# Attention's lead-in, first iteration and drain in orders of their own, 0/1 matrices by large instructions, and experts and last stage in one block

## The reference

```python
def _attn_ref(r, k, v, w, a, b) -> np.ndarray:
    B, H, S, D = r.shape
    state = np.zeros((B, H, D, D), dtype=np.float32)
    y = np.zeros_like(r)
    for t in range(S):
        ...
        y[:, :, t] = np.einsum('bhd,bhde->bhe', rt, state)
        Sa = np.einsum('bhde,bhe->bhd', state, at)
        state_decay = state * wt[:, :, None, :] - np.einsum('bhd,bhe->bhde', Sa, bt)
        state = state_decay + np.einsum('bhd,bhe->bhde', vt, kt)
    return y.astype(np.float32)

def _moe_ref(x, w_gate, w_noise, noise, w1, w2) -> np.ndarray:
    ...
    noisy_logits = logits + noise_scale * noise
    top2 = np.argpartition(-noisy_logits, 2, axis=1)[:, :2]
    ...
            h = np.maximum(x[mask] @ w1[e], 0.0)
            out[mask] += top2_w[mask, k, None] * (h @ w2[e])
    return out.astype(np.float32)

def _moe2_ref(x, w_in, w_out) -> np.ndarray:
    h = x @ w_in
    sp = np.where(h > 20.0, h, np.log1p(np.exp(np.minimum(h, 20.0))))
    g = h * np.tanh(sp)
    return (g @ w_out).astype(np.float32)
```

## Time and profile before

| | us |
|---|---|
| median of 3 runs (1692.13 to 1694.26) | 1694.13 |
| the profiled execution, whole | 1690.76 |
| its span | 1689.0 |

### The profile page before, as it was taken

One profiled execution on the slowest core, in us unless ns is written; L12 is line 12 of the kernel. 1 busy time (PEld: TensorE's weight loads), 2 busy tenths in 40 slices (PEclk: granted clock), 3 DMA queues, 4 the chain that ended last, 5 costly groups with the idle time before them and its releaser, 6 DMA issues. The chain is left out here.

```text
span 1689.0 us, 43070 instructions
## 1 busy us (share of the span) xinstructions
PE 1474.6 (87%) x18793; PEld 1138.5 (67%) x18793; DVE 597.6 (35%) x1198; ACT 575.3 (34%) x1137; POOL 326.6 (19%) x311
## 2 busy tenths in 40 slices
PE   0687897988989772699999999999858999999999
PEld 0577787877878661588888888888624555555556
DVE  8563653636544317000000000000027455454441
ACT  0453543525435310111111121212117545545541
POOL 5433222232321005311111111111041010000000
PEclk9877978969778755799999999999969999999999
DMA  3324133241321107555555555555161010000000
GB/s 85 81 52 112 39 87 70 53 114 38 90 67 27 43 19 251 181 186 164 187 164 185 167 179 172 173 175 171 45 196 30 24 31 28 24 28 9 8 12 20
DMA packets 99896, 159.88 MB, mean 95 GB/s; under 512 B 54464, under 2 KB 68800, under 8 KB 98432
## 3 DMA queue, kind: packets, MB, share of 16 engines
q1 hardware_dynamic: 92128, 131.23, 26.5%
q0 software_dynamic: 7584, 25.90, 5.0%
HBM read 140.21 MB, written 16.88 MB: 93 GB/s over the span
## 5 line engine op out<-in xcount | busy, mean ns | idle before, releaser
L951 PE MATMUL pY<-down,hT 128*128 x880 | 245.9, 433 | 0.0
L932 PEld LDWEIGHTS pH<-exT,up 128*128 128x128 f32 x1760 | 206.5, 193 | 11.5 <-issue 1.7
L1097 PE MATMUL mpY<-wout,h 128*128 128x320 f32 x768 | 210.4, 433 | 0.0
L932 PE MATMUL pH<-exT,up 128*128 128x128 f32 x1760 | 207.0, 276 | 2.5 <-ACT exT L971 1.5
L987 DVE COPY ys<-pY 128x320 f32<-128x320 f32 x55 | 27.0, 492 | 505.9 <-PE pY L951 505.9
L951 PEld LDWEIGHTS pY<-down,hT 128*128 128x128 f32 x880 | 163.0, 190 | 61.2
L978 ACT ACTIVATE hT<-pH 128x512 f32<-128x512 f32 x110 | 59.7, 594 | 418.0 <-PE pH L937 418.0
L1097 PEld LDWEIGHTS mpY<-wout,h 128*128 128x128 f32 x768 | 144.3, 190 | 60.7 <-issue 3.0
L1084 PE MATMUL mpH<-mxT,win 128*128 128x512 f32 x384 | 174.0, 607 | 4.9 <-ACT mxT L1126 4.1
L1084 PEld LDWEIGHTS mpH<-mxT,win 128*128 128x128 f32 x384 | 74.4, 195 | 92.6 <-issue 84.2
L1134 ACT ACTIVATE act_in<-act_in 128x512 f32<-128x512 f32 x96 | 59.9, 629 | 184.0 <-DVE act_in L1173 184.0
(11 more groups left out here) (179 smaller groups left out, 2196.8 us busy)
## 6 DMA issues: line engine op xcount, KB each, us to landing
up<-in_moe_w SPq DMA_DIRECT2D x55, 1024.0 KB
up_rest<-in_moe_w SPq DMA_DIRECT2D x110, 128.0 KB
down<-in_moe_w SPq DMA_DIRECT2D x8, 1280.0 KB, 14.6
results<-ys POOLq DMA_DIRECT2D x55, 160.0 KB
wfr<-in_wdec SPq DMA_DIRECT2D x16, 480.0 KB
kbT<-in_kb SPq DMA_DIRECT2D x16, 480.0 KB
uv<-in_vt SPq DMA_DIRECT2D x16, 240.0 KB, 6.2
aT<-in_at SPq DMA_DIRECT2D x16, 240.0 KB
```

What stands on the lines that cost most here:

```text
L932: pe.matmul(pH[t % 2][b][:, c, :], up[t % NU][:, k, f * P:(f + 1) * P], xT[t % 2][:, k, :], start=(c == 0 and k == 0), stop=False, skip_gr ...
L951: m = pe.matmul(pY[t % 2][:, 0:D], hT[t % 2][:, j, :], down[:, bass.ds(e, 1), j, :].rearrange("q n d -> q (n d)"), start=(j == 0), stop=(j ...
L1097: m = pe.matmul(pY[t % 2][:, 0:D], h[g % 2][:, f, j * P:(j + 1) * P], wout[:, f, :], start=(f == 0), stop=(f == FT - 1))
```

## The change

- In attention the list is chosen by iteration: LEAD in iteration 0, ORDER in 1 to 7, DRAIN in 8, SECOND_HALF in 9. LEAD begins with p0 and has the decays of group 1 (p0, p1), K, T, M and B at other places; DRAIN has the same operations as were left of ORDER, at other places between the hops.
- At the start VectorE clears `wfr` in two halves, makes the masks before the decays, and scales one half of group 0's `aT` and `kbT`, GpSimd the other; ScalarE clears the PSUM tiles. `wfr` is loaded in halves, each with its semaphore, and v of group 0 behind `kbT`.
- In routing VectorE marks tiles and rows with six large instructions in bf16, and ScalarE weights the tile matrix (2 large and 24 small instructions); GpSimd's 48 products and VectorE's 96 small instructions go.
- `experts` and `mish_ffn` return what each engine does, and `build` runs both in one block. The last stage's tiles `h` and two of `act_in` lie in the room of the down weights, its PSUM tiles are those of the experts, and its weights have room of their own. Its bodies are otherwise the same.

```diff
+
+LEAD = """p0 N0 K1 N1 K0 T0 M1 T1 n2_0 M0 n2_1 B0 t2_0 t2_1 w2_1 n4_0 w2_0 p1 n4_1 B1 t4_1 t4_0 V1 n8_0 w4_0 t8_1 t8_0
+w8_0 n8_1 n16_0 w4_1 n16_1 w16_0 w8_1 V0 L0 w16_1 E0 E1 L1 F0 F1""".split()
+DRAIN = """u s ST1 r u s r u UT1 s r H1 u s r u s r u s r u s I1 r J1 Y1 u UT0 s r H0 u X1 s r u ST0 s I0 r J0 Y0 u s
+X0 r u""".split()
 CHAIN = ("u", "s", "r")
 FIRST_HALF = ("UT0", "ST0", "H0", "I0", "J0", "Y0", "X0")
-SECOND_HALF = ("UT1", "ST1", "H1", "I1", "J1", "Y1", "X1")
+SECOND_HALF = ("ST1", "UT1", "H1", "I1", "J1", "Y1", "X1")
...
 
+    def order_of(it):
+        return LEAD if it == 0 else ORDER if it < GR else DRAIN if it == GR else SECOND_HALF
+
...
+        def scale_a(unit, eng, g, i):
+
+            eng.wait_ge(a_loaded, (g + 1) * 32)
+            eng.wait_ge(decayed, 2 * g + i + 1)
+            unit.tensor_tensor(aT[g % 3][:, i, :], aT[g % 3][:, i, :], dec[g % 3][i][:], ALU.mult).then_inc(a_scaled, 1)
+
+        def scale_kb(unit, eng, g, i):
+
+            eng.wait_ge(kb_loaded, (g + 1) * 32)
+            eng.wait_ge(decayed, 2 * g + i + 1)
+            backwards = after[i][:, ::-1].rearrange("q (c f) -> q c f", f=C).unsqueeze(2).to_broadcast([P, NC, 2, C])
+            unit.tensor_tensor(kbT[:, i], kbT[:, i], backwards, ALU.mult).then_inc(kb_scaled, 1)
+
         block = ctx.enter_context(nc.Block())
 
         @block.sync
         def _(sp):
-            def load_decays(g):
+            def load_decays(g, i):
                 for h in range(2):
-                    sp.dma_start(wfr[64 * h:64 * h + D], wdec[g, h]).then_inc(w_loaded, 16)
+                    sp.dma_start(wfr[64 * h:64 * h + D, i], wdec[g, h][:, i]).then_inc(w_loaded[i], 16)
...
 
-            sp.wait_ge(w_pads, 1)
-            load_decays(0)
-            load_v(0)
+            for i in range(2):
+                sp.wait_ge(w_pads, i + 1)
+                load_decays(0, i)
             sp.wait_ge(pads_set, 1)
             load_a(0)
             sp.wait_ge(pads_set, 2)
             load_kb(0)
+            load_v(0)
             sp.dma_start(gw[:], gate_w).then_inc(gate_loaded, 16)
             sp.wait_ge(pads_set, 3)
             for it in range(GR + 2):
                 g = it + 1
                 if g < GR:
-                    sp.wait_ge(decayed, 2 * it + 2)
-                    load_decays(g)
+                    for i in range(2):
+                        sp.wait_ge(decayed, 2 * it + i + 1)
+                        load_decays(g, i)
                 if 1 <= it <= GR:
                     if it >= 2:
...
+            act.wait_ge(zeros, 1)
+            for t in (*slot, chain):
+                m = copy(t[:].rearrange("q i w -> q (i w)"), st[:].rearrange("q c i f -> q (c i f)")[:, 0:2 * 512])
+            m.then_inc(cleared, 1)
             for it in range(GR + 2):
                 hop = 0
-                for tok in ORDER:
+                for tok in order_of(it):
...
             def make_decays(g, i):
-                dve.wait_ge(w_loaded, (g + 1) * 32)
...
-            nc.vector.memset(wfr[:], 1.0).then_inc(w_pads, 1)
-            for t in (mark, mark_r, st):
-                nc.vector.memset(t[:], 0.0)
-            for t in (*slot, chain):
-                m = nc.vector.memset(t[:], 0.0)
-            m.then_inc(cleared, 1)
-            dve.wait_ge(cleared, 1)
+            for i in range(2):
+                nc.vector.memset(wfr[:, i], 1.0).then_inc(w_pads, 1)
+            nc.vector.memset(st[:], 0.0).then_inc(zeros, 1)
+            nc.vector.memset(mark[:], 0.0)
+            after_step(nc.vector.memset(mark_r[:], 0.0))
             after_step(nc.vector.memset(mark_r[:, 0::C], 1.0))
-            make_decays(0, 0)
-            make_decays(0, 1)
             dve.wait_ge(const, 2)
             nc.vector.tensor_copy(identh[:], ident[:])
             for lo in (0, 64):
@@ -647,9 +658,15 @@
             dve.wait_ge(masked, 1)
             nc.vector.tensor_scalar(mask_un[:], mask_u[:], -1.0, None, ALU.mult).then_inc(masked, 1)
             dve.wait_ge(masked, 2)
+            make_decays(0, 0)
+            make_decays(0, 1)
+
+            dve.wait_ge(decayed, 2)
+            scale_a(nc.vector, dve, 0, 1)
+            scale_kb(nc.vector, dve, 0, 1)
             for it in range(GR + 2):
                 hop = 0
-                for tok in ORDER:
+                for tok in order_of(it):
                     if tok in ("p0", "p1"):
...
-            for j in range(2 * T):
-                nc.gpsimd.tensor_scalar(tile_hot[:, j, 1, :], minus_m[:], minus_tile[:, j // 2, j % 2:j % 2 + 1], row_of[:],
-                                        ALU.is_equal, ALU.mult).then_inc(by_pool, 1)
+            nc.gpsimd.tensor_copy(iota_rowh[:], iota_row[:])
+            nc.gpsimd.tensor_copy(minus_mh[:], minus_m[:]).then_inc(const, 1)
...
             for j in range(2 * T):
-                pe.wait_ge(by_dve, j + 1)
-                pe.wait_ge(by_pool, j + 1)
+                if j % QUARTER == 0:
+                    pe.wait_ge(in_row, j // QUARTER + 1)
+                if j % 2 == 0:
+
+                    pe.wait_ge(weighted, j // HALF + j // 2 + 2)
...
             nc.scalar.activation(gsum[:], gap[:], ACT.Exp).then_inc(soft, 1)
+            for half in range(2):
+                js = slice(half * HALF, (half + 1) * HALF)
+                act.wait_ge(in_tile, half + 1)
+                nc.scalar.activation(tile_hot[:, js, 1, :], tile_one[:, js, :], ACT.Copy, scale=row_of[:]).then_inc(weighted, 1)
+                for t in range(half * HALF // 2, (half + 1) * HALF // 2):
+                    nc.scalar.activation(tile_hot[:, 2 * t:2 * t + 2, 0, :], tile_one[:, 2 * t:2 * t + 2, :], ACT.Copy, scale=float(t)).then_inc(weighted, 1)
 
         @block.vector
...
             then(vec.scalar_tensor_tensor(minus_tile[:], row[:], 0.0, tile_f[:], ALU.is_lt, ALU.subtract))
-            vec.scalar_tensor_tensor(row[:], minus_tile[:], float(P), posf[:], ALU.mult, ALU.add).then_inc(split_up, 1)
-            dve.wait_ge(split_up, 1)
-            for j in range(2 * T):
-                vec.tensor_scalar(tile_hot[:, j, 0, :], minus_m[:], minus_tile[:, j // 2, j % 2:j % 2 + 1], float(j // 2), ALU.is_equal, ALU.mult)
-                vec.tensor_scalar(row_hot[:, j, :], iota_row[:], row[:, j // 2, j % 2:j % 2 + 1], None, ALU.is_equal).then_inc(by_dve, 1)
+            then(vec.scalar_tensor_tensor(row[:], minus_tile[:], float(P), posf[:], ALU.mult, ALU.add))
+
+            def mark_tiles(half):
+                js = slice(half * HALF, (half + 1) * HALF)
+                vec.tensor_tensor(tile_one[:, js, :], minus_mh[:].unsqueeze(1).to_broadcast([P, HALF, M]),
+                                  minus_tile[:].rearrange("q t k -> q (t k)")[:, js].unsqueeze(2).to_broadcast([P, HALF, M]), ALU.is_equal).then_inc(in_tile, 1)
+
+            def mark_rows(quarter):
+                js = slice(quarter * QUARTER, (quarter + 1) * QUARTER)
+                vec.tensor_tensor(row_hot[:, js, :], iota_rowh[:].unsqueeze(1).to_broadcast([P, QUARTER, P]),
+                                  row[:].rearrange("q t k -> q (t k)")[:, js].unsqueeze(2).to_broadcast([P, QUARTER, P]), ALU.is_equal).then_inc(in_row, 1)
+
+            mark_tiles(0)
+            mark_rows(0)
+            mark_tiles(1)
+            for quarter in range(1, 4):
+                mark_rows(quarter)
             then(vec.tensor_copy(pos[:].rearrange("q (t k) -> q t k", k=2), posf[:]))
...
 
-def experts(nc, x, results, w1, down, down_loaded, tile_expert, slot_token, ident):
...
+    return (load, gather, multiply, activate, combine), y_copied, pX, [p for tile in pH for p in tile], pY
...
+def mish_ffn(nc, ctx, results, results_copied, last, w_in, w_out, out, pos, gates, ident, room, pX, pH, pY):
...
+
+    GATE, ROWS = GT * GT * P, FT * GT * P
+    act_in = [room[:, 2 * ROWS + i * GATE:2 * ROWS + (i + 1) * GATE].rearrange("q (f n) -> q f n", n=GT * P) for i in range(2)]
+    act_in.append(sb("act_in", [P, GT, GT * P])[:])
+    h = [room[:, i * ROWS:(i + 1) * ROWS].rearrange("q (f n) -> q f n", n=GT * P) for i in range(2)]
+    pH = [p[:].rearrange("q c f -> q (c f)") for p in pH]
...
+                pe.wait_ge(wout_loaded, 16)
+                pe.wait_ge(results_copied, last)
...
         route(nc, logits, moe_noise, pos, gates, tile_expert, slot_token, ident, load_down)
-        experts(nc, x, results, moe_w1, down, down_loaded, tile_expert, slot_token, ident)
-        stage.close()
-        mish_ffn(nc, results, moe2_w_in, moe2_w_out, out, pos, gates, ident)
+        run_experts, results_copied, pX, pH, pY = experts(nc, stage, x, results, moe_w1, down, down_loaded, tile_expert, slot_token, ident)
+        run_ffn = mish_ffn(nc, stage, results, results_copied, M, moe2_w_in, moe2_w_out, out, pos, gates, ident,
+                           down[:].rearrange("q e t d -> q (e t d)"), pX, pH, pY)
+        block = stage.enter_context(nc.Block())
+
+        @block.sync
+        def _(sp):
+            run_experts[0](sp)
+            run_ffn[0](sp)
```

(20 more changed lines are left out.)

592 lines of the change are left out of this document (283 added, 309 removed).

## The result

The changed kernel takes 1655.59 us (median of 4 runs, 1650.57 to 1660.92) where the kernel before takes 1693.13 (4 runs beside it, 1691.86 to 1694.26): 37.5 us faster by the medians. The forecast was 1652.5 with a range of 1640 to 1664. The total was right; of its four terms two were right (routing and seam), the one for the lead-in was wrong, and the drain's is within the scatter.

What follows compares the result with a forecast made beforehand. Experts and last stage were taken as full on TensorE, so gains lie where TensorE waits: -13.3 (start and lead-in) + 3.4 (drain) - 18.9 (routing) - 12.8 (seam) = -41.6; 1694.1 - 41.6 = 1652.5 us, range 1640 to 1664.

Steps and rivals of the forecast that it cites:

- Start: Kernel start: kbT scaled at 25.6 us, first matmul 13 us sooner, but N0's mask only at 39.5 (before 40.28).
- Lead-in: Attention's iteration 0: first matmul of iteration 1 at 72.2 us, 13.3 us gained; bounds 9 and 17.
- B1 filled at 56.1: Lead-in: B1 filled at 56.1 us, then 16.1 us until kbT of group 1 is loaded and scaled, giving 72.2.
- F1 done at 66: Lead-in: at roughly 1 us per operation F1 is done at 66 us, before group 1's kbT at 72.2.
- Drain: Attention's drain: new order takes 55.1 us where 51.7 stood, 3.4 us lost; bounds 8 gained and 7 lost.
- never full, 7 lost: Drain's lower bound: if the granted clock is never full, the new order loses 7 us.
- Routing: Routing: inverse read at 664.7 us instead of 683.58 with matrices made by VectorE and ScalarE; 18.9 us gained.
- Rival 3: Routing: 0/1 matrices made slowly, broadcast operand at 2.1 ns per element; kernel at 1662 us; chance 0.07.
- Seam: Between experts and last stage: 12.8 us gained, 9.4 from the block's end and 3.4 from gathers not sharing queues.
- Rival 2: Seam: the wait stays because the stores' completion, not the block, took 9 us; kernel at 1661 us; chance 0.10.
- the first matmul near 72: Sign that the forecast is right: first matmul of attention's iteration 1 comes near 72 us.
- an iteration period off 70.5 by over 1.5 us: Sign that the forecast is wrong: attention's iterations differ from 70.5 us by over 1.5 us.

Runs made afterwards that it cites:

- late_loads: Changed kernel, but SyncE issues the loads of iteration 1 only behind N1 of group 1; 1649.0 us, ratio 0.9690 to the kernel before.
- route_only: Kernel before with only the new making of the routing's 0/1 matrices; 1678.38 us, ratio 0.9889.
- early_late_filler: Changed kernel with group 1's decays loaded before the clears' wait, iteration 1's loads behind N1, four unused matmuls behind each drain hop; 1633.56 us.

## Why the prediction was right, and where it was not

1. **Start.** Right by mechanism: the first matmul at 26.9 (25.6), p0 ahead of N0's mask, held by its load, that by the clears. The mask came at 40.74, forecast 39.5. The load took 4.7 us from issue where I had 5.2, but kbT was in at 21.7 where I had 20.5, and GpSimd's half of it took 4.99 beside VectorE's instruction where this chain had 3.4.
2. **Lead-in: the step that failed.** "B1 filled at 56.1" and kbT ready at 72.2 were right (55.6, 71.7). "F1 done at 66 ... F1 is no longer what comes last" was wrong: TensorE was in the list until 82.8, and the first matmul behind it came at 80.1 to 83.7 in all five traces with this lead-in and these loads. Two things were left out. One is the gaps: 10.8 us, of which 7.7 go with the loads. The row that warned stood in the trace of before; I had left it out because there it was hidden behind kbT:

```profile
76.03 0.66 PE L389 MATMUL wide<-tpow,npow 64*64 64x64 bf16 x27 [2.77 <-issue]
```

The other is in the sum itself. Behind B1 the list has 22 operations, which at the 1 us a step that the prediction names end near 78, not at 66. VectorE alone has p1's scans (until 59.31 here) and then ten takes of 0.96 us, so 66 couldn't be. `late_loads`, with 3.1 us of gaps, is through the list near 73, still after its kbT (70.3): the list came last even there. So 13.3 us forecast are 1.8 us at the first matmul of iteration 1 (83.71 against 85.47), and 3.1 at kbT of group 2 as a mean of three traces each (134.4 and 131.3).
3. **Drain.** +3.4 forecast, -1.3 by eleven traces, within their scatter. The direction of the argument (places matter little, the clock much) holds. The size was off at both ends: the 51.7 us of before were a short drain (51.9 to 60.4 from first to last u in the four traces of the old order, mean 56.0), and the new one came out below its 55.1 (48.5 to 54.6 in seven traces, mean 52.1). The bound "never full, 7 lost" doesn't follow from its own sum either: 60.4 less 51.7 is 8.7.
4. **Routing.** -18.9 forecast, -19.6 measured, each of the new instructions within 0.15 us. Rival 3 is out.
5. **Seam.** -12.8 forecast, -13.2 measured, and -13.4 for experts and seam together over all traces: 9.9 for the block's end (9.4) and 3.35 for the gathers (3.4). Rival 2 is out: GpSimd passed on 2.3 us behind the last store.
6. **Sum.** With routing and seam at 33 us, 4.5 of the measured 37.5 are attention's, where 9.9 were forecast. By the ratio (41.8), and by the medians of the second chip (42.1), it is 9. The total held because the two steady terms carry three quarters of it and more; attention's part is right in sign, its size can't be told (4.5 us by one estimate, 11 to 23 by another), and that it may come near 9.9 is luck, since the lead-in's 13.3 isn't there. Where that part arises when the lead-in gives only 1.8 to 3 us stays open: the rest lies in iterations and drain, which vary by more than that from run to run.

The prediction also took 0.2% (3.4 us) for what a measurement can tell from no change. The runs before it happened to agree; over 45 runs the kernel before took 1674 to 1710 us, and the intervals of the ratios above reach 6 to 11 us to either side, so a term of 3.4 us was out of reach.

Of the signs that I had named the first matmul near 72 didn't come, and one was badly chosen: "an iteration period off 70.5 by over 1.5 us" would have fired on the old attention, too: its iterations took 68.0 to 73.7 us in `route_only`.

## What to carry to other kernels

When a wait for data goes away, look at what was hidden in it: waits of the engine "for nothing" cost nothing inside a data wait and the full length outside, and here two of them were three and four times as long while data loads filled the queues (2.45 and 5.15 us against 0.82 and 1.30). Before a sum is made against one profile, ask which pieces repeat: here each piece outside attention repeated within 2.4 us and attention varied by 8 to 12. Look also for a load that waits for a clear it doesn't need: moving one wait down brought kbT of group 2 11.1 us forward, where the whole new lead-in had brought 3.1.

## What the runs showed of the hardware

- TensorE's waits at fixed places of its instruction stream: 0.8 to 1.3 us in `late_loads` with the DMA engines nearly idle (share 0.03 over the stretch), 2.5 to 5.2 in the changed kernel with them at 0.68 to 0.78; one of 3.31 at 0.07 in `early_late_filler`.
- The granted clock was kept by small matmuls in TensorE's gaps (1.00 through 42 us of drain), but once down it stayed at 0.50 through 31 us of which TensorE was busy 30.58, fillers included, before it rose.
- The kernel before took 1674 to 1710 us over 45 runs on three chips (1688 to 1710 over 23 on one of them), in step with its mean clock.
- The end of a block behind GpSimd's own stores: 9.9 us, and the same in every kernel that had it (first gather 12.2 to 12.6 us behind the last store, 2.3 without).
